# A delta-rule attention loop: values fetched ahead of the stores, and the last norm group one pass later

## The reference, cut to what matters

```python
k_n = k / (np.linalg.norm(k, axis=-1, keepdims=True) + 1e-06)
for t in range(S):                                   # S = 768, B = 4, H = 8, D = 48
    y[:, :, t] = einsum('bhd,bhde->bhe', q[:, :, t], state)
    v_old = einsum('bhde,bhd->bhe', state, k_n[:, :, t])
    state = state + bt * einsum('bhd,bhe->bhde', k_n[:, :, t], v[:, :, t] - v_old)
x = y laid out as 3072 tokens x 384
h = x @ w_in;  x = elu(h) @ w_out                    # 384 -> 2048 -> 384
# then gates with noise, the two best of 8 experts, each 384 -> 1024 -> 384 with a relu
```

## Time and profile before

| what | value |
|---|---|
| median of 3 runs | 1171.85 us (1170.71 to 1172.2) |
| profiled execution | 1170.71 us, of which the span is 1169.0 us |
| mean granted TensorE clock | 0.997 |
| PE busy | 1125.1 us (96%) |
| DVE busy | 647.1 us (55%) |
| ACT busy | 462.4 us (40%) |
| POOL busy | 355.5 us (30%) |

### The profile page before, as it was taken

One profiled execution on the slowest core, in us unless ns is written; L12 is line 12 of the kernel. 1 busy time (PEld: TensorE's weight loads), 2 busy tenths in 40 slices (PEclk: granted clock), 3 DMA queues, 4 the chain that ended last, 5 costly groups with the idle time before them and its releaser, 6 DMA issues.

```text
span 1169.0 us, 29044 instructions
## 1 busy us (share of the span) xinstructions
PE 1125.1 (96%) x11562; PEld 1070.6 (92%) x11562; DVE 647.1 (55%) x1552; ACT 462.4 (40%) x1048; POOL 355.5 (30%) x378
## 2 busy tenths in 40 slices
PE   5898999899999999999999999999999999999996
PEld 3886787688999999999999999999999999999995
DVE  5988788663455646465565647533534343434342
ACT  2236665684333333333333345423333333333331
POOL 4289995542002021020202012322222232322223
PEclk9999999999999999999999999999999999999998
DMA  7444555855997011110101011472424242424221
GB/s 158 132 124 100 123 127 141 219 165 196 368 360 244 21 46 41 37 41 20 41 20 41 14 51 65 172 230 73 168 75 171 77 167 85 157 93 148 62 70 53
DMA packets 82603, 137.30 MB, mean 117 GB/s; under 512 B 11050, under 2 KB 70034, under 8 KB 81466
## 3 DMA queue, kind: packets, MB, share of 16 engines
q1 hardware_dynamic: 68490, 87.97, 25.7%
q0 software_dynamic: 12992, 28.75, 7.6%
q10 hardware_dynamic: 1008, 18.97, 4.3%
HBM read 81.96 MB, written 53.77 MB: 116 GB/s over the span
## 4 chain that ended last, share of the span: by engine, by line
PE 74%; DVE 1%; issue 0%; ACT 0%; POOL 0%; ACTq 0%; POOLq 0%
PE ps_x L1403 18%; PE ps_x L1493 18%; PE ps_h L1392 17%; PE ps_h L1471 17%; PE ps_r L1451 2%; PE ps_r L1442 2%; DVE hg L1811 0%; ACT hg L1601 0%; POOL out_dram L1358 0%; DVE w_parts L1774 0%; PE ps_r L1510 0%; DVE x_raw L1804 0%; PE ps_r L1420 0%; ACT yT_d L1619 0%; PE ps_r L1418 0%
## 5 line engine op out<-in xcount | busy, mean ns | idle before, releaser
L1493 PE MATMUL ps_x<-hg,w_parts 128*128 128x400 f32 x1152 | 230.3, 346 | 0.0
L1403 PE MATMUL ps_x<-w_parts,hg 128*128 128x400 f32 x1152 | 229.6, 346 | 0.0
L1392 PE MATMUL ps_h<-xg,w_parts 128*128 128x384 f32 x1152 | 222.3, 338 | 0.0
L1471 PE MATMUL ps_h<-xg,w_parts 128*128 128x400 f32 x1116 | 220.6, 345 | 1.1 <-DVE w_parts L1774 1.1
L1403 PEld LDWEIGHTS ps_x<-w_parts,hg 128*128 128x128 f32 x1152 | 209.6, 188 | 0.0
L1811 DVE SCALAR_TENSOR_TENSOR hg<-ps_h,hg 128x400 fp32r<-128x400 f32 x128 | 73.6, 575 | 243.3 <-ACT hg L1601 242.8
L1392 PEld LDWEIGHTS ps_h<-xg,w_parts 128*128 128x128 f32 x1152 | 204.0, 188 | 2.5 <-DVE elu_parts L1668 2.5
L1471 PEld LDWEIGHTS ps_h<-xg,w_parts 128*128 128x128 f32 x1116 | 202.7, 188 | 4.0 <-issue 3.1
L1493 PEld LDWEIGHTS ps_x<-hg,w_parts 128*128 128x128 f32 x1152 | 206.1, 188 | 0.0
L1338 POOL DMA_INDIRECT xs_scratch<-x,rows_now x48 | 49.4, 1028 | 393.4 <-DVE rows_now L1748 293.9
L1601 ACT ACTIVATE hg<-ps_h 128x400 fp32r<-128x400 f32 x128 | 64.6, 505 | 256.5 <-PE ps_h L1471 256.5
(11 more groups left out here) (175 smaller groups left out, 1310.0 us busy)
## 6 DMA issues: line engine op xcount, KB each, us to landing
xs_scratch<-pads SPq DMA_DIRECT2D x2, 5502.0 KB, 42.1
x_rows<-xs_scratch SPq DMA_DIRECT2D x17, 614.1 KB
kqT<-in_kqT_dram SPq DMA_DIRECT2D x48, 192.0 KB, 4.0
carried<-in_w_dram ACTq DMA_DIRECT2D x3, 3072.0 KB, 11.2
w_raw<-in_w_dram ACTq DMA_DIRECT2D x3, 3072.0 KB, 11.0
xs_scratch<-pads SPq DMA_DIRECT2D x6, 1375.5 KB, 16.7
out_dram<-pads SPq DMA_DIRECT2D x1, 4800.0 KB, 30.5
xs_scratch<-pads SPq DMA_DIRECT2D x6, 786.0 KB, 8.9
```

The costliest lines, as they stand in the source:

```text
L1392: mm = nc.tensor.matmul(ps_h[f % 2][:, 0:TB], wi[:, a, k, f * P:(f + 1) * P], xr[:, b, k, :], start=(i == 0), stop=(i == len(passes) - 1))
L1403: mm = nc.tensor.matmul(ps_x[t][:, 0:DG], act_r[:, f % RING, a, t * P:(t + 1) * P], wo[:, b, f, :], start=(f == 0 and i == 0), stop=(f == ...
L1471: mm = nc.tensor.matmul(ps_h[f % 2][:, 0:TR], w1, xg[:, b, k, :], start=(m == 0), stop=(m == len(passes) - 1))
L1493: mm = nc.tensor.matmul(ps_y[k][:, 0:TR], w2r[i][:, a, s, k * P:(k + 1) * P], hg[:, s % RING, b, :], start=(s == 0 and m == 0), stop=(s == ...
```

## The change

It has three parts, all in the attention loop.

- On SP both `load_v` of a pass, for chunks 2m+4 and 2m+5, go to the head of the pass, ahead of `store(2m-2)`. Before, each stood behind a store, a `load_kqT` and a `load_k`.
- On SP each weight piece goes directly behind its store, ahead of `load_kqT`. The third piece of a pass stays at its end.
- On DVE and ACT the preparation of group 2 is moved: set 4 is turned at the end of pass 0 instead of ahead of the loop, set 5 at the end of pass 1 instead of pass 0 and with it `square_norms(2)`; the root and the gains come in pass 2 instead of pass 1. `place(2, 0)` moves from the middle of pass 7 to the end of pass 6. POOL's table is the same.

```diff
@@ SP, the loop over passes
             for m in range(PAIRS):
+                for n in (2 * m + 4, 2 * m + 5):
+                    if n < NIT:
+                        load_v(n)
                 pieces = ...
                 for n in (2 * m - 2, 2 * m - 1):
                     if m:
                         store(n)
+                        for i in pieces[n % 2:n % 2 + 1]:
+                            load_weights(i)
                         if n + DEEP < NIT:
                             sp.wait_ge(y_done, n + 1)
                             load_kqT(n + DEEP)
                         if n + K_DEEP < NIT - B:
                             load_k(n + K_DEEP)
-                    if n + DEEP < NIT:
-                        load_v(n + DEEP)
-                    for i in pieces[n % 2:n % 2 + 1]:
-                        load_weights(i)
@@ ACT
-                if m == 1:
+                if m == 2:
                     root_of(2)
@@ DVE
-            to_set_lanes(2, (4,))
             for m in range(PAIRS):
...
-                if m == 1:
+                if m == 2:
                     invert_root(2)          # divide_by_root(2), refine_root(2) likewise
...
-                if m == 7:
-                    place(2, 0)
                 residuals(a, 2)
...
-                if m == 0:
-                    to_set_lanes(2, (5,))
-                    square_norms(2)
+                if m < 2:
+                    to_set_lanes(2, (4 + m,))
                 if m == 1:
+                    square_norms(2)
+                if m == 2:
                     gains(2)
                     turn_norms(2)
                 if m == 4:
                     place(1, 1)
-                if m == 7:
-                    place(2, 1)
+                if m in (6, 7):
+                    place(2, m - 6)
```

More of the change, by code:

```diff
@@ L997, in _ @@
                     mask_products(b + 2, 1)
-                if m == 0:
-                    to_set_lanes(2, (5,))
+                if m < 2:
+                    to_set_lanes(2, (4 + m,))
+                if m == 1:
                     square_norms(2)
-                if m == 1:
+                if m == 2:
                     gains(2)
```

## The result

The changed kernel takes 1181.33 us (median of 4 runs, 1180.02 to 1182.08), the kernel before 1171.8. The ratio is 1.0082, with an interval of [1.0064, 1.0099]: slower by 9.5 us. The forecast was slower by 5.3 us, to 1177.1 us, with a range of 1172.3 to 1182.0. The direction and the first part of the mechanism held; the size was 4.2 us too small. The result lies outside the forecast's own 1174.2 to 1180 and next to rival 3's 1180.4; it is inside the stated range by 0.7 us, and a second measurement of the same kernel (f11, 1183.63 us) is not. The profiled execution of after took 1187.28 us (span 1185.5, clock 0.991). It is the longest of eight executions (1179.42 to 1187.28), so its losses are larger than those of the median.

A forecast was written before the change was run, and what follows sets the result against it. PE is always busy behind the attention, so attention delays move the end; inside it POOL is full to 190 us. Pass 7's 7.8 - 1.1 - 1.4 = +5.3 us gives 1176.0 for the profiled execution, median 1177.1, range 1172.3 to 1182.

The forecast's parts named there:

- rival 3: SP's queue slower than the rows, POOL's slip at its upper bound, ACT waiting for stores; 1180.4 us, 20 in 100.
- POOL's slip: Delay s of POOL's columns and later scalings while it waits for group 2's gains in pass 2; 6.0 us, bounds 4.3 to 7.6.
- The chain: End of pass 2, from the start of group 2's gains to POOL's scaling; 1.44 us, as for group 1.
- the mask's shift: How much later DVE's last mask of pass 2 starts; between 0 and 2.5 us, taken as 1.7.
- The keys in pass 2: Keys and queries of chunk 6 reach PE at 112.2 instead of 110.71; 1.5 us late.
- The way through SP: From POOL's two scalings through value loads, store and key issue to the keys' landing; 9.5 us.
- chunk 16 in pass 7: Its keys and queries arrive at 198.1 against 190.34, so pass 7 runs 7.8 us late, earlier chunks' delays included.
- my formula: A chunk's keys arrive at POOL's scaling start plus 9.5 us plus s; lateness is against PE's old reading time.
- No new delay there: From pass 7 on POOL has no columns and value loads fill SP's former waiting time, so nothing is added.
- What comes back: Savings: -1.1 us from place(2, 0) leaving the middle of pass 7, and -1.4 us from ACT's weight wait in pass 8.
- The weights' -1.4: In pass 8 ACT's 1.91 us wait for the second weight piece shrinks; -1.4 us, bounds 0 and -1.9.
- PE's unexplained idle time: 3.8 us without releaser in passes 8 and 9; change taken as 0, bounds -3.8 and +3.8.

The follow-up runs named there:

- f11: The changed kernel again, unchanged, for a second profiled execution in another batch; 1183.63 us, ratio 1.0099 against the kernel before.
- e4: The changed kernel with keys and queries of chunk 2m+4 issued at the head of SP's pass, ahead of both value loads; 1180.58 us, ratio 1.0063.
- e7: The changed kernel with the loads of values 2 and 3 ahead of the loads of keys before the loop; 1179.19 us, ratio 1.0063.
- f10: The changed kernel with values 2 and 3 loaded before the keys ahead of the loop, plus ten idle products in passes 2, 5 and 6; 1179.5 us, ratio 1.0062.
- f9: The changed kernel with ten idle matrix products on PE ahead of the products of keys in passes 2, 5 and 6; 1182.02 us, ratio 1.0096.
- e5: The changed kernel with ten idle matrix products on PE ahead of the products of keys in passes 2 and 6; 1184.44 us, ratio 1.0106.
- e2: The kernel before with only the preparation of group 2 moved one pass later on DVE and ACT; 1176.9 us, ratio 1.0033.
- e1: The kernel before with only both value loads moved to the head of SP's pass; 1174.71 us, ratio 1.0024.
- e3: The kernel before with only each weight piece moved directly behind its store; 1173.21 us, ratio 1.0005.

## Why the prediction was right, and what it mis-sized

- *POOL's slip.* Forecast s = 6.0 with an upper bound of 7.6, measured 8.0 (8.9 in f11, from ACT's first output). The way of working it out holds better than its result. In every profile with the norms moved POOL scales group 2 at 30.3 to 31.0 us after the first output plus the delay of the loop by chunk 3: after 33.9 - 3.6 = 30.3, f11 34.9 - 4.6 = 30.3, e4 33.3 - 3.0 = 30.3, e7 29.2 + 1.1 = 30.3, f10 30.5 - 0.2 = 30.3, f9 32.8 - 2.0 = 30.8, e5 32.6 - 1.8 = 30.8, e2 33.0 - 2.0 = 31.0. In the kernel before it scaled at 26.0. So s is 4.3, the forecast's lower bound, plus the loop's delay in pass 2. The chain (1.44) was exact. The term that failed was the mask's shift, taken as 1.7 and in truth 3.7 (from 27.55 to 31.30 us after the first output), because the keys were later than forecast.
- *The keys in pass 2.* Forecast 1.5 us late, measured 4.5. From POOL's start (105.30) to PE's products (116.61) it was 11.3 us and not 9.5, and PE was there 1.2 us earlier against the first output (112.07 - 98.03 = 14.0, before 110.71 - 95.44 = 15.3). That makes 1.5 + 1.8 + 1.2. The last of these I had written down myself, as the 1.0 us of norm steps saved in pass 1, and had not set against the keys.
- *The way through SP.* The rows of pass 5 above: values to values 1.54 as forecast, values to store 2.78 instead of 1.78, store to keys 1.11, issue of the keys to PE's products 5.31 instead of 4.15. Rival 3 had the slower queue, at 20 in 100, and with it a slip at the upper bound and ACT's wait for a store: all three came, and its sum, 1180.4, is the nearest to the 1181.33 measured. It too had no term for the clock.
- *The end of the columns' passes.* I named chunk 16 in pass 7. The loss came at chunks 12 and 14, in passes 5 and 6, and by pass 7 the loop was so late that chunk 16 was in time. That the delays don't add, since each is measured against POOL, is what e1 shows. By my formula chunk 14 had to be 166.6 + 9.5 + 6.0 - 174.7 = 7.4 us late (166.6 is 167.50 less a scaling's 0.83; PE read chunk 14 at 174.68 in the trace of before). In after it was (188.76 - 98.03) - (174.68 - 95.44) = 11.5. The 4.1 more are the slip's 2.0 and the way's 2.1 (11.6 from 177.16 to 188.76, instead of 9.5).
- *The clock.* Not in the forecast, and what it costs can be read from PE. Take the delay against before when PE begins the products that had waited, and the delay of the next output in the table (chunk 3 for pass 2, 9 for pass 5, 11 for pass 6):

  | profile and pass | wait for keys | clock behind it | delay at the products | at the next output |
  |---|---|---|---|---|
  | after, 5 | 2.64 | full | 7.2 | 7.2 |
  | f11, 6 | 0.64 | full | 10.8 | 10.8 |
  | f9, 5 | 0.51 | full | 6.3 | 6.3 |
  | f9, 6 | 0.99 | full | 9.8 | 9.8 |
  | f10, 6 | 0.61 | full | 7.2 | 7.2 |
  | e1, 2 | 5.18 | half | 6.3 | 7.8 |
  | f11, 5 | 3.08 | half | 8.6 | 10.1 |
  | e7, 5 | 2.80 | half | 2.6 | 4.2 |
  | e7, 6 | 2.40 | half | 6.6 | 8.2 |
  | e5, 5 | 2.74 | half | 6.0 | 8.9 |
  | after, 6 | 3.96 | half | 11.5 | 14.4 |

  At full clock the delay does not grow behind the wait; at half clock it grows by 1.5 to 2.9 us. Pass 2 adds 0.3 us in after and 1.4 in f11, so in these passes the clock costs 3.2 of after's 13.9 us and 2.9 of f11's 13.5. The rest is the waits themselves. Holding the clock with idle products (f9, f10) moved the medians by -1.6 us in one batch and by +0.3 us between two chips, with the products' own time in it. So the clock's part is shown in the profiles and not resolved in the medians.
- *The right sides.* "No new delay there" was said of the time from pass 7 on. In after it held but for 1.0 us (12.9 at chunk 15, 13.9 at chunk 23), in f11 it did not (10.7, then 13.5). And I had not looked at DVE's `right_side` in passes 1 to 5, which waits for POOL's scaled values; e2 shows it, 3.0 us at once.
- *What comes back.* `place(2, 0)`: forecast -1.1; the delay shrinks by 1.0 from chunk 11 to 13 in after, e2, e4 and e7, 0.7 in f11 and 0.4 in f9; in f10 it grows by 0.9, behind a wait of 1.91 us for the keys of chunk 16. The weights' -1.4 did not come (e3). PE's unexplained idle time grew by 2.6 us in e3 and is 3.6 us in after (2.2 + 0.8 + 0.6).
- *The parts.* Values 0.24, norms 0.33, weights 0.05 per cent make 0.62; the whole is 0.82 (0.99 in f11). The interval of after reaches down to 0.64, and each part's own is 0.14 to 0.16 wide to either side, so an interplay of the parts isn't certain; it would fit that late keys lengthen the slip.

The step-by-step signs asked for were there: the wait on POOL's scaling, PE's waits in passes 2, 5 and 6 (not 7), no wait of ACT for weights in pass 8, the network unchanged. These were not: the last column at 195.9 (it was 200.4, or 197.8 without the later beginning), ACT's output of pass 7 near 197.9 (207.18, or 204.6), the network later by 5 us (13.9, without the later beginning), and pass 7 at 15.7 us (16.65).

What stays open: why PE's idle time without a releaser moves with the weights' loads, and how much of the 8 us between executions of e7 comes from POOL's start, which I saw only in profiled executions.

## What to carry to other kernels

When an engine has no slack and no place in the period, price an edit by asking when that engine gets its input, and then follow each of its products to all of its readers: here keys, stores and right sides all hung on POOL, and taking one of them out of the way (e4) gained 2 to 4 us of 10 by the medians, within their intervals. Before a load that waits is moved ahead of others in a queue, add up everything behind it, and take the slower of the rows for each issue and each landing, because now several transfers are in flight together. A consumer that gets faster by the same edit makes a late load later: set both shifts against each other.

## What the runs showed of the hardware

- PE's granted clock fell to half behind waits of 2.40 (e7), 2.74 (e5), 2.80 (e7), 3.08 and 4.11 (f11), 3.96 and 4.54 (after) and 5.18 us (e1) for keys, and behind 2.66 and 3.13 (e2) and 3.00 us (e4) for DVE. It stayed full behind 2.64 (after), 1.91 (f10) and 1.31 us (e5). The 16 products of a chunk then took up to 1.97 us instead of 1.08, if the fall came before or in them.
- Idle products in the wait kept it at 1.00 from 100 to 260 us (f9, f10), with no gain that the medians can tell.
- Behind such a wait the loop lost another 1.5 to 2.9 us where the clock was at half, and nothing in five cases where it was full (the table above).
- A chain of small DVE instructions runs faster when POOL stands still: the last of the gains of group 2 took 0.22 or 0.23 us in all eight profiles in which POOL waited for it, and 0.60 to 1.03 us in the six in which POOL was busy (0.84 in before).
- SP issues two rows of keys and queries in 0.92 to 2.35 us in the loop of one and the same trace (after), and the keys took 4.2 to 5.5 us from their issue to PE's products when values and a store had gone just ahead, where the median landing was 3.7.
